# A fused convolution and two expert layers on one core: GpSimd takes two of the weight splits, and a factor of 2 pi changes its place

## The chip, the cores and the metric

The kernel runs on one core of one Trainium2 chip. TensorE multiplies, VectorE (DVE) and ScalarE (ACT) work on tiles in SBUF and PSUM, GpSimd (POOL) does nothing but four small constants in this kernel, and SyncE issues nearly all the DMAs. The metric is device microseconds of one execution. Before the change the median of three runs is 2252.99 us (2252.92 to 2253.04).

## The reference, cut to what matters

```python
w = exp(weight - max);  w = w / (sum(w) + 1e-9)                 # 8 heads, 7 taps
out = np.einsum('hk,bskhg->bshg', w, x_unf)                     # causal 7-tap filter, 4 x 4096 tokens, 192 channels
h = x @ w_in;  g = h * np.cos(h);  x = g @ w_out                # layer one, 192 -> 2048 -> 192
h = np.maximum(x @ w_in, 0.0);  return h * h @ w_out            # layer two, the same sizes
```

Everything is float32 in and out.

## The kernel before, in words

The 16384 tokens are worked in 32 tiles of 512. For each tile VectorE makes the seven taps (`conv`), TensorE multiplies up from 192 channels to 2048 (`h`, in pairs of 128 rows, so eight pairs per tile and layer), ScalarE and VectorE make the activation `g`, and TensorE multiplies down into `y`. Layer one is called A, layer two B. A turn `i` of the program has 16 slots: the eight pairs of A of tile `i` and the eight of B of tile `i - 1`, in the order of the table `SLOTS` (the first turn has only the A pairs, `FIRST_SLOTS`). In each slot TensorE does the up products of that slot's pair together with the down products of the pair four slots earlier (`LAG`).

Each factor is split into a high part, rounded to the multiplier's format, and a low part that holds the rest: three products (low by high, high by low, high by high) stand for one of float32. So the weights too exist as `_hi` and `_lo`. High parts are written by ScalarE (`down_hi_main`, L514, and `down_hi_side`, L518, for the down weights), low parts by VectorE by subtracting the high part from the staged float32 weights (L663 for layer one, L678 for layer two). The staged down weights of both layers lie in one buffer, `late`, one after the other: the second layer's load waits until the first layer's low parts are made. 128 of the 192 output channels are the main ones (`dn_hi`, `dn_lo`), 64 the side ones (`dn_side`, which holds both parts).

Layer one's `h` is divided by 2 pi when it is read (L528), so that the cosine can be taken of turns: L686 and L688 take off the whole turns, L537 is the sine with a quarter turn added, L694 multiplies. What is missing, a factor of 2 pi, is in the down weights of layer one: `scale=TWO_PI` at L514 and L518, and the multiplication in L663.

Which instruction stands where is written by hand. In the first turn VectorE does `layer1_down_lo` in slots 3 and 4 (its pairs A0 and A1), ScalarE the high parts in the same slots; the tables `LATE_AT` and `LATE_LOW_AT` put the second layer's weights at later slots: ScalarE's `dn_hi_B` at slot 8 of the first turn, VectorE's `dn_lo_B` and `dn_side_B` at slot 2 of the second turn. TensorE waits for low parts before the first down products of A (`down_waits`), and for those of B a turn later. `FILL` puts eight products on zeros before two of the first turn's last down steps.

`read_y1` (L554, L555, ScalarE) and `split_y1` (L729 to L738, VectorE) read `y_A` from PSUM once per tile and make layer two's input of it.

Of the kernel before, what the change touches and what calls it, by code (L numbers as in the profile page):

```python
# [17 lines left out]
ALU = mybir.AluOpType  # L18
ACT = mybir.ActivationFunctionType
F32 = mybir.dt.float32  # L20
# [3 lines left out]
P = 128  # L24
# [93 lines left out]
def tile_program(nc, x, taps_in, w1i, w1o, w2i, w2o, out):  # L118
# [15 lines left out]
    with ExitStack() as ctx:  # L134
# [72 lines left out]
        wi_lo = sem("wi_lo")  # L207
        late_hi_made = sem("late_hi_made")
        late_lo = sem("late_lo")
        even_made = sem("even_made")  # L210


# [41 lines left out]
        @block.sync  # L254
        def _(sp):
            def load_x(t):
                sp.dma_start(xt[:, :], x[t]).then_inc(x_loaded, 16)

            def load_layer1_up(part, a, b):
                sp.dma_start(stage_in[:, a:b], w1i[0:P, a:b]).then_inc(wi_loaded[part], 16)  # L260
                for half in (top, low):
                    sp.dma_start(stage_in_side[half, a:b], w1i[P:D, a:b]).then_inc(wi_loaded[part], 16)

            def store_y(t):
                sp.wait_ge(y2_copied, t + 1)
                sp.dma_start(out_tiles[t, 0:P, :], yt).then_inc(y_stored, 16)
                sp.wait_ge(y2_summed, t + 1)
                sp.dma_start(out_tiles[t, P:D, :], yt_side).then_inc(y_stored, 16)

            def load_layer2_up(half):  # L270
                cols = slice(half * HALF, (half + 1) * HALF)
                sp.dma_start(stage_main, w2i[0:P, cols]).then_inc(up2_loaded, 16)
                for rows in (top, low):
                    sp.dma_start(stage_side[rows, :], w2i[P:D, cols]).then_inc(up2_loaded, 16)

            def load_down(weights):
                sp.dma_start(stage_out, weights.rearrange("p (c d) -> p c d", d=D)).then_inc(down_loaded, 16)

            load_x(0)
            load_layer1_up(0, 0, FIRST_PART)  # L280
            load_layer1_up(1, FIRST_PART, F)
            load_down(w1o)
            sp.wait_ge(tap_done, K)
            load_x(1)
            sp.wait_ge(wi_lo, 4)
            load_layer2_up(0)
            sp.wait_ge(late_lo, 2)
            load_down(w2o)
            sp.wait_ge(tap_done, 2 * K)
            load_x(2)  # L290
            sp.wait_ge(late_lo, 4)
            sp.wait_ge(even_made, 1)
            load_layer2_up(1)

            sp.wait_ge(tap_done, 3 * K)
            load_x(3)
            for i in (2, 3):
                store_y(i - 2)
                sp.wait_ge(tap_done, (i + 2) * K)
                load_x(i + 2)  # L300
            with sp.Fori(4, TILES - 2) as i:
                store_y(sp.snap(i - 2))
                sp.wait_ge(tap_done, sp.snap((i + 2) * K))
                load_x(sp.snap(i + 2))
            for t in range(TILES - 4, TILES):
                store_y(t)
            sp.wait_ge(y_stored, 32 * TILES)

        @block.tensor
        def _(pe):  # L310
# [4 lines left out]
            def up_waits(turn, s, kind, p):  # L315
                freed = turn.before(s, HB)
                if freed:
                    pe.wait_ge(taken[freed[0]], freed[1])
                if p == 0 and kind == "A":
                    pe.wait_ge(x1_hi, 3 * (turn.i + 1))  # L320
                    pe.wait_ge(x1_made, turn.i + 1)
                if p == 0 and kind == "B":
                    pe.wait_ge(x2_made, turn.i)
                if turn.peeled and turn.i == 0 and p in (0, 2):
                    pe.wait_ge(wi_lo, 2 + p)
                if turn.peeled and turn.i == 1 and p == 0 and kind == "B":
                    pe.wait_ge(late_lo, 4)
                    pe.wait_ge(even_made, 1)
                if turn.peeled and turn.i == 1 and p == NP // 2 and kind == "B":
                    pe.wait_ge(late_lo, 8)  # L330
                    pe.wait_ge(even_made, 2)

            def up_step(turn, s, kind, p, rows, k):
# [26 lines left out]

            def down_waits(turn, kind, p, back):
                if turn.peeled and turn.i - back == 0 and p == 0:
                    pe.wait_ge(late_lo, 2)
                if turn.peeled and turn.i - back == 1 and p == 0 and kind == "B":
                    pe.wait_ge(late_lo, 6)
                if kind == "B" and p == 0 and turn.runs("O") and not turn.last(kind, back):
                    pe.wait_ge(y2_copied, turn.i - 1)
                    pe.wait_ge(y2_summed, turn.i - 1)
                if fine(turn, p):
                    pe.wait_ge(hi_made[kind], turn.count(kind, p, back))  # L370
                else:
                    pe.wait_ge(lo_made[kind], turn.count(kind, p, back))
# [109 lines left out]
        def _(act):  # L482
# [26 lines left out]
                act.activation(up_even[hi_rows["B"], half, :], even[:, :, 0, :], ACT.Copy).then_inc(even_made, 1)  # L509

            def down_hi_main(k):

                act.wait_ge(down_loaded, {"A": 16, "B": 32}[k])
                act.activation(dn_hi[k][:, :, :], stage_out[:, :, 0:P], ACT.Copy,  # L514
                               scale={"A": TWO_PI, "B": 1.0}[k]).then_inc(late_hi_made, 1)

            def down_hi_side(k):
                act.activation(dn_side[k][:, :, 0:SIDE], stage_out[:, :, P:D], ACT.Copy,  # L518
                               scale={"A": TWO_PI, "B": 1.0}[k]).then_inc(late_hi_made, 1)

            def read_h(turn, s, kind, p):
                act.wait_ge(filled[kind], turn.count(kind, p))
# [24 lines left out]
            def read_y1(turn, back):  # L547

                act.wait_ge(down_low["A"][0], turn.count("A", NP - 1, back))
                act.wait_ge(down_top["A"][1], turn.count("A", NP - 1, back))  # L550
                if back and turn.runs("B", 1):
                    act.wait_ge(filled["B"], turn.count("B", NP - 1, 1))
                x_hi = layer_in(turn, "B", back - 1)[0]
                act.activation(y_side[top, :], y["A"][low, 1, :], ACT.Copy).then_inc(y1_copied, 1)  # L554
                act.activation(x_hi[:, :], y["A"][:, 0, :], ACT.Copy).then_inc(y1_copied, 1)  # L555

            def read_y2(turn):
                count = turn.count("B", NP - 1, 1)
# [69 lines left out]
        def _(dve):  # L628
# [25 lines left out]
                dve.tensor_tensor(up_lo["A"][:, a:b], stage_in[:, a:b], up_hi["A"][:, a:b].bitcast(F32),  # L654
                                  ALU.subtract).then_inc(wi_lo, 1)

            def layer1_down_lo(m):
                dve.wait_ge(late_hi_made, m + 1)
                if m == 0:
                    lo, staged, hi = dn_lo["A"][:, :, :], stage_out[:, :, 0:P], dn_hi["A"][:, :, :]  # L660
                else:
                    lo, staged, hi = dn_side["A"][:, :, SIDE:], stage_out[:, :, P:D], dn_side["A"][:, :, 0:SIDE]
                dve.scalar_tensor_tensor(out=lo, in0=staged, scalar=TWO_PI, in1=hi.bitcast(F32), op0=ALU.mult,  # L663
                                         op1=ALU.subtract).then_inc(late_lo, 1)

            def late_lo_part(n):
                if n in (1, 3):
                    cols = slice(n // 2 * HALF, (n // 2 + 1) * HALF)
                    parts = ((up_lo["B"][:, cols], stage_main, up_hi["B"][:, cols]),
                             (up_side["B"][hi_rows["B"], cols], stage_side[hi_rows["B"], :],  # L670
                              up_side["B"][hi_rows["B"], cols]))
                else:
                    parts = ((dn_lo["B"][:, :, :], stage_out[:, :, 0:P], dn_hi["B"][:, :, :]),
                             (dn_side["B"][:, :, SIDE:], stage_out[:, :, P:D], dn_side["B"][:, :, 0:SIDE]))
                for m, (lo, staged, hi) in enumerate(parts):

                    dve.wait_ge(late_hi_made, 2 * n + 1 + m)
                    dve.tensor_tensor(lo, staged, hi.bitcast(F32), ALU.subtract).then_inc(late_lo, 1)  # L678

            def fraction(turn, r, p):  # L680
# [44 lines left out]
            def split_y1(turn, back):  # L725
                n = turn.i + 1 - back
                x_hi, x_lo, x_side, x_side_lo = layer_in(turn, "B", back - 1)
                dve.wait_ge(y1_copied, n * 2 - 1)
                dve.tensor_tensor(y_side[top, :], y["A"][top, 1, :], y_side[top, :], ALU.add)\  # L729
                   .then_inc(x2_step, 1)  # L730
                dve.wait_ge(x2_step, n * 2 - 1)
                dve.tensor_copy(x_side[low, :], y_side[top, :])
                dve.tensor_copy(x_side[top, :], y_side[top, :]).then_inc(x2_step, 1)
                dve.wait_ge(y1_copied, n * 2)
                dve.tensor_tensor(x_lo[:, :], y["A"][:, 0, :], x_hi[:, :].bitcast(F32),
                                  ALU.subtract)
                dve.wait_ge(x2_step, n * 2)
                dve.tensor_tensor(x_side_lo[lo_rows["B"], :], y_side[top, :],  # L738
                                  x_side[top, :].bitcast(F32), ALU.subtract).then_inc(x2_made, 1)
# [8 lines left out]
            def body(turn):  # L748
# [10 lines left out]
                for s, (kind, p) in enumerate(turn.slots()):  # L759
# [16 lines left out]
                            tap(turn, k)  # L776
                    if kind == "A" and turn.runs("A"):
                        fraction(turn, s % RING, p)
                    if turn.peeled and turn.i == 0 and kind == "A" and p < 2:
                        layer1_down_lo(p)  # L780
                    if turn.peeled and (turn.i, s) in LATE_LOW_AT:
                        late_lo_part(LATE_LOW_AT[turn.i, s])

            turns(dve, body)


# [40 lines left out]
```

## Time and profile before

| | |
|---|---|
| median of 3 runs | 2252.99 us |
| the profiled execution | 2253.41 us |
| its span | 2251.1 us |
| TensorE matmul busy | 2239.1 us (99%) |
| VectorE busy | 1774.6 us (79%) |
| ScalarE busy | 1734.8 us (77%) |
| GpSimd busy | 0.2 us, 4 instructions |
| mean granted TensorE clock | 0.999 |

The span runs from the first to the last instruction of the trace; 2.3 us of the profiled execution's time lie around it. Busy shares are means over the whole; TensorE is busy nearly all the time, so what matters is where in the program it is not, and what it waits for there. Chains and waits of the profile name for each instruction what released it last.

### The profile page before, as it was taken

What the parts mean: (1) busy time and instruction counts of PE and PEld (TensorE: products, weight loads), DVE (VectorE), ACT (ScalarE), POOL (GpSimd) and SP (SyncE); (2) the same over time, 40 slices, a digit from 0 to 9 for tenths busy, and PEclk for the clock granted to TensorE, in tenths of its full rate; (3) what the DMA queues carried; (4) which work ended last, traced back from release to release, by engine and by line L of the source; (5) the groups of instructions that cost most, each with busy time, mean ns of one, the idle gap of its engine ahead of it and who ended that gap; (6) DMA issues with size and microseconds to landing.
All of it is one profiled execution on the core that took longest, in us unless ns stands there. A gap on an engine that the chain in (4) does not pass through costs nothing.

```text
span 2251.1 us, 46857 instructions
## 1 busy us (share of the span) xinstructions
PE 2239.1 (99%) x19526; PEld 2213.3 (98%) x19526; DVE 1774.6 (79%) x1813; ACT 1734.8 (77%) x1844; POOL 0.2 (0%) x4
## 2 busy tenths in 40 slices
PE   8999999999999999999999999999999999999999
PEld 7899999999999999999999999999999999999998
DVE  8887788777787777887778877778877788777773
ACT  6677777777877777777778777787777787777876
POOL 0000000000000000000000000000000000000000
PEclk9999999999999999999999999999999999999999
DMA  4000000000000000000000000000000000000000
GB/s 127 27 15 15 9 14 12 10 14 7 14 14 7 14 9 13 14 7 14 14 7 14 14 7 14 7 14 14 7 14 14 7 14 14 7 14 7 7 8 15
DMA packets 13456, 33.26 MB, mean 15 GB/s; under 512 B 1905, under 2 KB 1905, under 8 KB 13169
## 3 DMA queue, kind: packets, MB, share of 16 engines
q1 hardware_dynamic: 13280, 32.81, 4.9%
q8 instruction: 24, 0.39, 0.1%
q14 instruction: 8, 0.06, 0.0%
q10 hardware_dynamic: 144, 0.00, 0.0%
HBM read 20.22 MB, written 12.58 MB: 15 GB/s over the span
## 4 chain that ended last, share of the span: by engine, by line
PE 97%; DVE 2%; ACT 1%; issue 0%; DMA 0%
PE h L346 10%; PE h L350 10%; PE h L348 10%; PE h L352 10%; PE y_A L402 5%; PE y_A L396 5%; PE y_A L400 5%; PE y_A L398 5%; PE y_A L404 5%; PE h L355 5%; PE y_B L400 5%; PE y_B L398 5%; PE y_B L396 5%; PE y_B L404 5%; PE y_B L402 5%; DVE conv L712 0%
## 5 line engine op out<-in xcount | busy, mean ns | idle before, releaser
L698 DVE TENSOR_TENSOR g_lo<-g,g_hi 128x1024 fp32r<-128x1024 f32 x512 | 625.2, 1221 | 272.0 <-ACT g_hi L545 271.1
L545 ACT ACTIVATE g_hi<-g 128x1024 fp32r<-128x1024 f32 x512 | 538.3, 1052 | 44.1 <-DVE g L694 43.4
L537 ACT ACTIVATE w<-w,quarter 128x1024 f32<-128x1024 f32 x256 | 295.5, 1154 | 304.6 <-DVE w L688 304.6
L396 PE MATMUL y_A<-g_hi,dn_lo_A 64*128 64x512 f32 x1024 | 396.9, 388 | 0.1
L402 PE MATMUL y_A<-g_hi,dn_side_A 64*128 64x512 f32 x1024 | 396.3, 387 | 0.0
L398 PE MATMUL y_A<-g_hi,dn_hi_A 64*128 64x512 f32 x1024 | 396.0, 387 | 0.0
L400 PE MATMUL y_A<-g_lo,dn_hi_A 64*128 64x512 f32 x1024 | 395.8, 387 | 0.0
L404 PE MATMUL y_A<-g_lo,dn_side_A 64*128 64x512 f32 x1024 | 395.8, 387 | 0.0
L348 PE MATMUL h<-x_hi_A,up_lo_A 64*128 64x512 f32 x1024 | 394.5, 387 | 0.0
L352 PE MATMUL h<-x_hi_A,up_hi_A 64*128 64x512 f32 x1024 | 394.5, 386 | 0.0
L350 PE MATMUL h<-x_lo_A,up_hi_A 64*128 64x512 f32 x1024 | 394.4, 386 | 0.0
L396 PE MATMUL y_B<-g_hi,dn_lo_B 64*128 64x512 f32 x1000 | 386.6, 387 | 0.0
L398 PE MATMUL y_B<-g_hi,dn_hi_B 64*128 64x512 f32 x1000 | 386.1, 386 | 0.0
L400 PE MATMUL y_B<-g_lo,dn_hi_B 64*128 64x512 f32 x1000 | 386.0, 386 | 0.0
L404 PE MATMUL y_B<-g_lo,dn_side_B 64*128 64x512 f32 x992 | 382.9, 386 | 0.0
L402 PE MATMUL y_B<-g_hi,dn_side_B 64*128 64x512 f32 x992 | 382.9, 386 | 0.0
L352 PE MATMUL h<-x_hi_B,up_hi_B 64*128 64x512 f32 x992 | 382.9, 386 | 0.0
L348 PE MATMUL h<-x_hi_B,up_lo_B 64*128 64x512 f32 x992 | 382.9, 386 | 0.0
L350 PE MATMUL h<-x_lo_B,up_hi_B 64*128 64x512 f32 x992 | 382.9, 386 | 0.0
L694 DVE TENSOR_TENSOR g<-w,g 128x1024 f32<-128x1024 f32 x256 | 313.7, 1225 | 22.7 <-ACT w L537 1.2
L688 DVE SCALAR_TENSOR_TENSOR w<-w,g 128x1024 f32<-128x1024 f32 x256 | 313.7, 1225 | 8.8
L528 ACT ACTIVATE g<-h 128x1024 f32<-128x1024 f32 x256 | 262.2, 1024 | 70.2 <-PE h L352 59.5
(122 smaller groups left out, 6180.0 us busy)
## 6 DMA issues: line engine op xcount, KB each, us to landing
xt<-x SPq DMA_DIRECT2D x32, 393.0 KB, 3.1
out<-late SPq DMA_DIRECT2D x32, 256.0 KB, 2.0
out<-late SPq DMA_DIRECT2D x32, 128.0 KB, 2.3
late<-w_out SPq DMA_DIRECT2D x2, 1536.0 KB, 9.5
stage_in_side<-w_in SPq DMA_DIRECT2D x2, 512.0 KB, 4.2
stage_in_side<-w_in SPq DMA_DIRECT2D x4, 256.0 KB, 5.3
w<-w_in SPq DMA_DIRECT2D x1, 768.0 KB, 7.1
stage_in_side<-w_in SPq DMA_DIRECT2D x2, 384.0 KB, 9.1
```

Of the source, the lines that this page charges most:

```text
L348: mm = pe.matmul(dst, up_lo[kind][rows, f], x_hi[rows, :], start=False, stop=z)
L350: mm = pe.matmul(dst, up_hi[kind][rows, f], x_lo[rows, :], start=False, stop=z)
L352: mm = pe.matmul(dst, up_hi[kind][rows, f], x_hi[rows, :], start=False, stop=z)
L396: mm = pe.matmul(sums[:, 0, :], dn_lo[kind][rows, c, :], hi, start=a, stop=False)
L398: mm = pe.matmul(sums[:, 0, :], dn_hi[kind][rows, c, :], hi, start=False, stop=False)
L400: mm = pe.matmul(sums[:, 0, :], dn_hi[kind][rows, c, :], lo, start=False, stop=z)
L402: mm = pe.matmul(sums[:, 1, :], dn_side[kind][rows, c, :], hi, start=a, stop=False)
L404: mm = pe.matmul(sums[:, 1, :], dn_side[kind][rows, c, :], lo, start=False, stop=z)
L545: act.activation(g_hi[:, s % RING, :, :], g[:, s % RING, :, :], ACT.Copy).then_inc(hi_made[kind], 1)
L688: dve.scalar_tensor_tensor(out=v, in0=v, scalar=ROUND, in1=u, op0=ALU.subtract, op1=ALU.subtract).then_inc(frac, 1)
L694: dve.tensor_tensor(u, v, u, ALU.mult).then_inc(g_made, 1)
L698: dve.tensor_tensor(g_lo[:, r, :, :], g[:, r, :, :], g_hi[:, r, :, :].bitcast(F32), ALU.subtract).then_inc(lo_made[kind], 1)
```

## The change

GpSimd gets a program of two subtractions, the low parts of the main channels of the down weights: `dn_lo_A` as soon as ScalarE has made `dn_hi_A`, `dn_lo_B` as soon as it has made `dn_hi_B`. VectorE no longer does them. A new semaphore `pool_lo` counts them, and the three places that waited for VectorE's `late_lo` wait for both. The 2 pi leaves the down weights of layer one and is applied where `y_A` is read: as a scale in ScalarE's two reads, and in VectorE's two instructions that read `y_A` from PSUM, which turn from `tensor_tensor` into `scalar_tensor_tensor`.

```diff
+        pool_lo = sem("pool_lo")
...
-            sp.wait_ge(late_lo, 2)
+            sp.wait_ge(late_lo, 1)
+            sp.wait_ge(pool_lo, 1)
             load_down(w2o)
...
                 if turn.peeled and turn.i - back == 0 and p == 0:
-                    pe.wait_ge(late_lo, 2)
+                    pe.wait_ge(late_lo, 1)
+                    pe.wait_ge(pool_lo, 1)
                 if turn.peeled and turn.i - back == 1 and p == 0 and kind == "B":
-                    pe.wait_ge(late_lo, 6)
+                    pe.wait_ge(late_lo, 4)
+                    pe.wait_ge(pool_lo, 2)
...
-                act.activation(dn_hi[k][:, :, :], stage_out[:, :, 0:P], ACT.Copy,
-                               scale={"A": TWO_PI, "B": 1.0}[k]).then_inc(late_hi_made, 1)
+                act.activation(dn_hi[k][:, :, :], stage_out[:, :, 0:P], ACT.Copy).then_inc(late_hi_made, 1)
...
-                act.activation(y_side[top, :], y["A"][low, 1, :], ACT.Copy).then_inc(y1_copied, 1)
-                act.activation(x_hi[:, :], y["A"][:, 0, :], ACT.Copy).then_inc(y1_copied, 1)
+                act.activation(y_side[top, :], y["A"][low, 1, :], ACT.Copy, scale=TWO_PI).then_inc(y1_copied, 1)
+                act.activation(x_hi[:, :], y["A"][:, 0, :], ACT.Copy, scale=TWO_PI).then_inc(y1_copied, 1)
...
-                dve.scalar_tensor_tensor(out=lo, in0=staged, scalar=TWO_PI, in1=hi.bitcast(F32), op0=ALU.mult,
-                                         op1=ALU.subtract).then_inc(late_lo, 1)
+                dve.tensor_tensor(dn_side["A"][:, :, SIDE:], stage_out[:, :, P:D],
+                                  dn_side["A"][:, :, 0:SIDE].bitcast(F32), ALU.subtract).then_inc(late_lo, 1)
...
-                dve.tensor_tensor(y_side[top, :], y["A"][top, 1, :], y_side[top, :], ALU.add)\
-                   .then_inc(x2_step, 1)
+                dve.scalar_tensor_tensor(out=y_side[top, :], in0=y["A"][top, 1, :], scalar=TWO_PI, in1=y_side[top, :],
+                                         op0=ALU.mult, op1=ALU.add).then_inc(x2_step, 1)
...
-                dve.tensor_tensor(x_lo[:, :], y["A"][:, 0, :], x_hi[:, :].bitcast(F32),
-                                  ALU.subtract)
+                dve.scalar_tensor_tensor(out=x_lo[:, :], in0=y["A"][:, 0, :], scalar=TWO_PI,
+                                         in1=x_hi[:, :].bitcast(F32), op0=ALU.mult, op1=ALU.subtract)
...
+        @block.gpsimd
+        def _(pool):
+            for k, made in (("A", 1), ("B", 5)):
+                pool.wait_ge(late_hi_made, made)
+                pool.tensor_tensor(dn_lo[k][:, :, :], stage_out[:, :, 0:P], dn_hi[k][:, :, :].bitcast(F32),
+                                   ALU.subtract).then_inc(pool_lo, 1)
```

VectorE, slots 3 to 5 of the first turn, before (each name is output, then inputs; `late` holds the staged down weights):

```order
L686 TENSOR_SCALAR w<-g 128x1024
L688 SCALAR_TENSOR_TENSOR w<-w,g 128x1024
L663 SCALAR_TENSOR_TENSOR dn_lo_A<-late,dn_hi_A 128x2048
L694 TENSOR_TENSOR g<-w,g 128x1024
L708 TENSOR_SCALAR conv<-xt,taps 128x768
L686 TENSOR_SCALAR w<-g 128x1024
L688 SCALAR_TENSOR_TENSOR w<-w,g 128x1024
L663 SCALAR_TENSOR_TENSOR dn_side_A<-late,dn_side_A 128x16x64
L698 TENSOR_TENSOR g_lo<-g,g_hi 128x1024
```

And the same place after the change:

```order
L683 TENSOR_SCALAR w<-g 128x1024
L685 SCALAR_TENSOR_TENSOR w<-w,g 128x1024
L691 TENSOR_TENSOR g<-w,g 128x1024
L705 TENSOR_SCALAR conv<-xt,taps 128x768
L683 TENSOR_SCALAR w<-g 128x1024
L685 SCALAR_TENSOR_TENSOR w<-w,g 128x1024
L661 TENSOR_TENSOR dn_side_A<-late,dn_side_A 128x16x64
L695 TENSOR_TENSOR g_lo<-g,g_hi 128x1024
```

One instruction has gone, the one on 128x2048, ahead of the first product with the cosine; the order of the others is as it was.

VectorE, slot 2 of the second turn, before:

```order
L694 TENSOR_TENSOR g<-w,g 128x1024 [waits cosine]
L678 TENSOR_TENSOR dn_lo_B<-late,dn_hi_B 128x2048 [waits late_hi_made]
L678 TENSOR_TENSOR dn_side_B<-late,dn_side_B 128x16x64 [waits late_hi_made]
L698 TENSOR_TENSOR g_lo<-g,g_hi 128x1024 [waits hi_made_A]
L686 TENSOR_SCALAR w<-g 128x1024 [waits taken_A]
```

After:

```order
L691 TENSOR_TENSOR g<-w,g 128x1024 [waits cosine]
L675 TENSOR_TENSOR dn_side_B<-late,dn_side_B 128x16x64 [waits late_hi_made]
L695 TENSOR_TENSOR g_lo<-g,g_hi 128x1024 [waits hi_made_A]
L683 TENSOR_SCALAR w<-g 128x1024 [waits taken_A]
L685 SCALAR_TENSOR_TENSOR w<-w,g 128x1024 [waits whole]
```

Here too the one on 128x2048 has gone.

GpSimd, its whole program after the change (before it ended with the fourth of the constants):

```order
L821 MEMSET const-float32-0.0 128x1
L821 MEMSET const-float32-1.0 128x1
L821 MEMSET const-bfloat16-1.0 128x1
L821 MEMSET const-uint8-127 128x1
L783 UNCONDITIONAL_BRANCH [waits barrier_Pool_Activation_PE_DVE_SP_gather]
L788 ISA
L788 TENSOR_TENSOR dn_lo_A<-late,dn_hi_A 128x2048 [waits late_hi_made]
L788 TENSOR_TENSOR dn_lo_B<-late,dn_hi_B 128x2048 [waits late_hi_made]
```

The second subtraction waits for the fifth high part, `dn_hi_B`, which ScalarE makes in slot 8 of the first turn: it stands some eight slots earlier in the program than VectorE's did.

## Rows read from the trace of the kernel before

**Rows 1.** The page's first part: busy time, share, instructions.

```profile
PE 2239.1 (99%) x19526; PEld 2213.3 (98%) x19526; DVE 1774.6 (79%) x1813; ACT 1734.8 (77%) x1844; POOL 0.2 (0%) x4
```

**Rows 2.** Waits after 82.1 us: engine, line, releaser: total us, times, longest.

```profile
ACT w L537 <- DVE w L688: 292.9, 245, 3.6
...
PE h L346 <- ACT g L530: 0.7, 1, 0.7
```

**Rows 3.** The chain that ended last, 16 to 50 us: start, us, what.

```profile
22.88 1.28 DVE dn_lo_A L663
...
24.99 1.22 DVE g L694
...
46.94 1.01 ACT g L528
...
48.00 0.50 PE h L346
```

**Rows 4.** VectorE in order of time, 16 to 83 us: start, us, what, idle before it.

```profile
21.65 1.23 DVE L688 SCALAR_TENSOR_TENSOR w<-w,g 128x1024 f32<-128x1024 f32 x1
22.79 2.29 DVE L663 SCALAR_TENSOR_TENSOR dn_lo_A<-late,dn_hi_A 128x2048 fp32r<-128x2048 f32 x1
...
30.05 1.22 DVE L698 TENSOR_TENSOR g_lo<-g,g_hi 128x1024 fp32r<-128x1024 f32 x1
...
51.00 1.22 DVE L698 TENSOR_TENSOR g_lo<-g,g_hi 128x1024 fp32r<-128x1024 f32 x1
...
56.24 1.22 DVE L698 TENSOR_TENSOR g_lo<-g,g_hi 128x1024 fp32r<-128x1024 f32 x1
...
82.20 2.29 DVE L678 TENSOR_TENSOR dn_lo_B<-late,dn_hi_B 128x2048 fp32r<-128x2048 f32 x1
```

**Rows 5.** ScalarE in order of time, 20 to 50 us.

```profile
20.52 1.90 ACT L514 ACTIVATE dn_hi_A<-late 128x2048 fp32r<-128x2048 f32 x1
22.91 1.15 ACT L537 ACTIVATE w<-w,quarter 128x1024 f32<-128x1024 f32 x1 [0.49 <-DVE w L688]
...
47.84 1.91 ACT L514 ACTIVATE dn_hi_B<-late 128x2048 fp32r<-128x2048 f32 x1
```

**Rows 6.** TensorE matmuls in order of time, 28 to 82 us.

```profile
28.24 0.39 PE L352 MATMUL h<-x_hi_A,up_hi_A 64*128 64x512 f32 x1
31.41 0.46 PE L346 MATMUL h<-x_side_lo,up_side_A 64*128 64x512 f32 x1 [2.79 <-DVE g_lo L698]
...
52.45 0.39 PE L396 MATMUL y_A<-g_hi,dn_lo_A 64*128 64x512 f32 x1
...
61.06 2.12 PE L455 MATMUL y_B<-x_side_last 128*128 128x512 f32 x8
...
66.09 0.39 PE L400 MATMUL y_A<-g_lo,dn_hi_A 64*128 64x512 f32 x1
66.64 0.47 PE L396 MATMUL y_A<-g_hi,dn_lo_A 64*128 64x512 f32 x1
...
82.00 0.50 PE L346 MATMUL h<-x_side_B,up_side_B 64*128 64x512 f32 x1 [0.70 <-ACT g L530]
```

**Rows 7.** TensorE by stretches: us, busy (matmuls), granted clock, DMA share, GB/s.

```profile
31.40:32.40 1.00, 0.99 (x8) 0.98 0.68 209
32.40:35.50 3.10, 3.10 (x17) 0.50 0.94 392
```

**Rows 8.** Groups by shape: line, operation, shapes, count, busy us, mean ns, idle before.

```profile
L729 DVE TENSOR_TENSOR y_side<-y_A,y_side 64x512 f32<-64x512 f32 x32 | 21.8, 682 | 99.5 <-ACT y_side L554 99.5
...
L528 ACT ACTIVATE g<-h 128x1024 f32<-128x1024 f32 x256 | 262.2, 1024 | 70.2 <-PE h L352 59.5
L530 ACT ACTIVATE g<-h 128x1024 f32<-128x1024 f32 x256 | 260.9, 1019 | 61.3 <-PE h L355 55.4
```

**Rows 9.** One tile's reading in the steady part: VectorE's last step, TensorE's first use.

```profile
209.26 0.68 DVE L738 TENSOR_TENSOR x_side_lo<-y_side,x_side_B 64x512 fp32r<-64x512 f32 x1
...
211.73 0.39 PE L346 MATMUL h<-x_side_B,up_side_B 64*128 64x512 f32 x1
```

More of the change, by code:

```diff
@@ L290, in _ @@
             load_x(2)
-            sp.wait_ge(late_lo, 4)
+            sp.wait_ge(late_lo, 3)
             sp.wait_ge(even_made, 1)
@@ L326, in up_waits @@
                 if turn.peeled and turn.i == 1 and p == 0 and kind == "B":
-                    pe.wait_ge(late_lo, 4)
+                    pe.wait_ge(late_lo, 3)
                     pe.wait_ge(even_made, 1)
                 if turn.peeled and turn.i == 1 and p == NP // 2 and kind == "B":
-                    pe.wait_ge(late_lo, 8)
+                    pe.wait_ge(late_lo, 6)
                     pe.wait_ge(even_made, 2)
@@ L513, in down_hi_main @@
                 act.wait_ge(down_loaded, {"A": 16, "B": 32}[k])
-                act.activation(dn_hi[k][:, :, :], stage_out[:, :, 0:P], ACT.Copy,
-                               scale={"A": TWO_PI, "B": 1.0}[k]).then_inc(late_hi_made, 1)
+                act.activation(dn_hi[k][:, :, :], stage_out[:, :, 0:P], ACT.Copy).then_inc(late_hi_made, 1)
             def down_hi_side(k):
-                act.activation(dn_side[k][:, :, 0:SIDE], stage_out[:, :, P:D], ACT.Copy,
-                               scale={"A": TWO_PI, "B": 1.0}[k]).then_inc(late_hi_made, 1)
+                act.activation(dn_side[k][:, :, 0:SIDE], stage_out[:, :, P:D], ACT.Copy).then_inc(late_hi_made, 1)
             def read_h(turn, s, kind, p):
@@ L655, in layer1_up_lo, with layer1_down_lo @@
                                   ALU.subtract).then_inc(wi_lo, 1)
[L657 to L662, printed above, removed]
-                dve.scalar_tensor_tensor(out=lo, in0=staged, scalar=TWO_PI, in1=hi.bitcast(F32), op0=ALU.mult,
-                                         op1=ALU.subtract).then_inc(late_lo, 1)
+            def layer1_down_lo():
+                dve.wait_ge(late_hi_made, 2)
+                dve.tensor_tensor(dn_side["A"][:, :, SIDE:], stage_out[:, :, P:D],
+                                  dn_side["A"][:, :, 0:SIDE].bitcast(F32), ALU.subtract).then_inc(late_lo, 1)
             def late_lo_part(n):
@@ L672, in late_lo_part @@
                 else:
-                    parts = ((dn_lo["B"][:, :, :], stage_out[:, :, 0:P], dn_hi["B"][:, :, :]),
-                             (dn_side["B"][:, :, SIDE:], stage_out[:, :, P:D], dn_side["B"][:, :, 0:SIDE]))
+                    parts = ((dn_side["B"][:, :, SIDE:], stage_out[:, :, P:D], dn_side["B"][:, :, 0:SIDE]),)
                 for m, (lo, staged, hi) in enumerate(parts):
-                    dve.wait_ge(late_hi_made, 2 * n + 1 + m)
+                    dve.wait_ge(late_hi_made, 2 * n + 1 + m + (n == 2))
                     dve.tensor_tensor(lo, staged, hi.bitcast(F32), ALU.subtract).then_inc(late_lo, 1)
@@ L778, in body @@
                         fraction(turn, s % RING, p)
-                    if turn.peeled and turn.i == 0 and kind == "A" and p < 2:
-                        layer1_down_lo(p)
+                    if turn.peeled and turn.i == 0 and kind == "A" and p == 1:
+                        layer1_down_lo()
                     if turn.peeled and (turn.i, s) in LATE_LOW_AT:
```

## The prediction

> **What bounds the kernel now.** I read the page's busy shares first, then the waits, the chain, and the first 90 us in order of time. TensorE is busy in 2239.1 of 2251.1 us [rows 1], so only work that TensorE waits for can matter. After 82.1 us the list of waits has one matmul wait, 0.7 us (the instruction at 82.00); all other waits there are of VectorE and ScalarE, above all 292.9 us of ScalarE for VectorE [rows 2]. That is slack: from 82.00 us the end is 82.00 plus TensorE's own work, and the change takes none of it away. The price is therefore read as the shift of that instruction.
>
> Before it, VectorE leads. The chain runs through VectorE's pair stream: `w` ends at 22.88, `dn_lo_A` follows, the cosine product starts at 24.99, and by way of the sine and the read of `h` it comes out at TensorE's slot at 48.00 [rows 3]. VectorE stands idle once between 21 and 60 us, for 0.26 us by my reading of its whole list; the rows kept are in [rows 4]. TensorE sits idle from 28.6 to 31.4, until the first `g_lo` [rows 6]. From 48.00 to 72 TensorE and VectorE run nearly in step: a `g_lo` comes every 5.24 us (51.00, 56.24) [rows 4], and TensorE's slot plus its eight products on zeros lasts as long. The down step alone that starts at 52.45 needs the `g_lo` that ends at 52.22: slack 0.23 us [rows 4, 6].
>
> **The change, part by part.**
>
> *`dn_lo_A` leaves VectorE.* The instruction lasts 2.29 us, but the next one, the cosine product, needs the sine, which ends at 22.91 + 1.15 = 24.06 [rows 5]. It can move from 24.99 to 24.1 at best: a gain of 0.9 us, and the wait for the sine is what is late next. All that follows on VectorE is in the same order, so the slot at 48.00 comes 0.9 us earlier.
>
> *`dn_lo_B` leaves VectorE.* It stood at 82.20 [rows 4], behind the last point where TensorE waits. The instructions behind it come sooner, and nobody waits for them: 0.
>
> *GpSimd's subtraction, alone.* No row shows GpSimd on a large tile. From below: VectorE's 2.29 us for the same shape [rows 4], one pass. From above: three passes, two reads and a write one after the other, 6.87 us. I take two passes, 4.58 us, since the instruction has two large inputs. The Trainium skill (GPSIMD Engine Reference, section 3.1) gives 4.497 us for this operation and size; with it each term below is 0.1 us smaller. As a mere producer GpSimd is in time: `dn_hi_A` is done at 20.52 + 1.90 = 22.42 [rows 5], and TensorE and the load of the second down weights need the result only behind the first `g_lo`, at 31.3 before and 30.4 with the gain. Even 6.87 us would end at 29.3. `dn_lo_B` starts after `dn_hi_B`, at 49.75, and is needed at about 91: 40 us of cover. If the first subtraction took over 8 us, that cover would be gone and TensorE would wait for `pool_lo`.
>
> *GpSimd beside VectorE.* The trace has no stretch with both at work in SBUF, so the ends are: fully beside each other (0 us), and fully one after the other, a VectorE instruction with two SBUF tiles waiting out the whole subtraction. I take the second end. It is the choice that decides the sign. The Trainium skill (SBUF — State Buffer, section Who interferes with whom) says that GpSimd reads through an interface which VectorE's second SBUF input also uses, and that whichever starts first blocks the other for its whole instruction; no run here shows it yet. By that rule the sum is the one that follows; without it the change is worth the 0.9 us.
>
> With exclusion, place by place. First subtraction: `w` (two inputs) is under way until 22.88, then VectorE would be waiting for the sine, so GpSimd gets in at 22.9 and ends at 22.9 + 4.58 = 27.5. The cosine product starts there and not at 24.99: +2.5 us, on the chain to 48.00. Everything queued behind it on VectorE moves with it, the first `g_lo` (30.05) [rows 4] and so the load of the second down weights too, which has ten microseconds to spare before `dn_hi_B` at 47.84 [rows 5]. Second subtraction: ready at 49.75 (+2.5), in the middle of VectorE's full stretch. It gets in between two of its instructions and holds up the `g_lo` of 51.00, or one of the next, by 4.58 us. TensorE's slack there is 0.23 [rows 4, 6]: +4.35 us. VectorE cannot catch up, since the products on zeros and its own 5.24 us period leave nothing.
>
> *The clock.* After the idle 2.8 us TensorE was granted 0.50, the 1.2 GHz level, from 32.4 to 35.5 [rows 6, 7], so 3.1 us gave half the work, and with the edges 1.6 us are lost. There it cost nothing: TensorE had slack in that slot. In the second stall TensorE stands 4.3 us and I expect the same drop, now where it and VectorE run in step. Slack before the last down step: 66.09 plus the cadence of 0.23 against 66.64, 0.3 us [rows 6]. So +1.3 us; from below 0, if the clock holds.
>
> *The 2 pi at the reading of y.* ScalarE's read with a scale costs what one without does (L528 1024 ns with 1/2 pi, L530 1019 without) [rows 8], and on SBUF tiles VectorE's two forms last the same (L663 and L678, 2.29 us each) [rows 4]. From PSUM the trace has only the plain form, 682 ns [rows 8]; between 0 and twice as long for two instructions is 0 to 1.4 us per tile. I take 0. In the steady part the reading ends at 209.94, and TensorE uses it at 211.73 [rows 9]: 1.8 us of cover hide even the upper end. Without that cover it would be 32 times the excess.
>
> **The sum.** 2.5 + 4.35 + 1.3 = 8.2 us. Against the profiled execution's own 2253.41 us (a span of 2251.1 and 2.3 around it) that is 2261.6, and against the median, 0.4 lower, 2261.2. I say 2261. With 2.29 us for the subtraction the terms are 0.2, 2.1 and 0 to 1.3: 2255.3 to 2256.6. With 6.87: 4.8, 6.65 and 1.3: 2265.7.
>
> **The rivals.**
>
> *No contention.* GpSimd works beside VectorE; only the 0.9 us of the first part show: 2252.1. Not slower. For it: the two engines are separate in every row, and the time VectorE waits for ScalarE (24.06 is fixed) bounds the gain. Against it: both read the same tile types from the same SBUF at the moment when VectorE runs without a pause. It decides from an overlap at which the cosine product starts before 24.99.
>
> *Sharing.* Both go on, each slowed. The first subtraction then overlaps VectorE from 24.06 to 27.5; at half speed VectorE loses 1.7 of that, less the 0.9: +0.8. The second costs half of 4.58, less 0.23: +2.1. Together 2255.9, too little to tell from no change. For it: memory traffic is often shared; against it: nothing in the trace has that shape.
>
> *GpSimd is too slow.* Over 8 us each, TensorE waits for `pool_lo`; with exclusion at 9 us the terms are 6.9, 8.8 and 1.3: 2270.
>
> *The change doesn't do what it says.* The work is the same and the instructions are in the program; I give that no chance.
>
> **How the numbers follow.** Exclusion 0.60, its own range 2256 to 2266; no contention 0.24; sharing 0.13; too slow 0.03. What a measurement can tell from no change is 0.2%, 4.5 us. A gain of 4.5 us would need five times the best the chain offers: faster 0.02. Same: 0.24 + 0.13, and 0.05 of the exclusion case with a short subtraction, less the 0.02: 0.40. Slower: 0.58. The range goes from just under the rival without contention to 2264, which leaves out the 0.02 and about 0.13 above.
>
> **What would show it.** In the changed profile: GpSimd's two subtractions with their durations near 4.6 us, the first from 22.9; a gap on VectorE ahead of the cosine product until the first one ends, or a cosine product at 24.1; a gap of the second one's length on VectorE near 52 to 60 us; TensorE idle in front of the down step after the slot at 50.5, and a granted clock of 0.5 behind it; the instruction that stood at 82.00 at about 90. The forecast is wrong if VectorE's instructions start during a subtraction, or if GpSimd's lasts under 3 us or over 7.

## The result, and the profile after

The changed kernel takes 2262.89 us (median of 6, 2260.59 to 2264.56) against 2253.01 us before (6 runs): a ratio of 1.0042, 95% interval 1.0032 to 1.0051. It is slower by 9.9 us; forecast were 2261 and a range of 2251.8 to 2264. The profiled execution took 2264.56 us, the longest of the six and above that range; its span is 2261.6, 10.5 more than before.

GpSimd's two subtractions in the changed kernel, in order of time (start, us, instruction, idle before it and releaser):

```profile
22.99 4.62 POOL L788 TENSOR_TENSOR dn_lo_A<-late,dn_hi_A 128x2048 fp32r<-128x2048 f32 x1 [22.54 <-ACT dn_hi_A L517]
52.30 4.57 POOL L788 TENSOR_TENSOR dn_lo_B<-late,dn_hi_B 128x2048 fp32r<-128x2048 f32 x1 [24.69 <-ACT dn_hi_B L517]
```

And VectorE beside them, same columns:

```profile
21.94 1.23 DVE L685 SCALAR_TENSOR_TENSOR w<-w,g 128x1024 f32<-128x1024 f32 x1
24.39 4.30 DVE L691 TENSOR_TENSOR g<-w,g 128x1024 f32<-128x1024 f32 x1 [1.22 <-ACT w L538]
...
32.53 1.22 DVE L695 TENSOR_TENSOR g_lo<-g,g_hi 128x1024 fp32r<-128x1024 f32 x1
...
52.33 5.62 DVE L685 SCALAR_TENSOR_TENSOR w<-w,g 128x1024 f32<-128x1024 f32 x1
57.88 1.21 DVE L695 TENSOR_TENSOR g_lo<-g,g_hi 128x1024 fp32r<-128x1024 f32 x1
```

The two VectorE instructions that start while a subtraction runs are not late in starting; they are long. Both last 1.22 us elsewhere (their groups mean 1237 and 1242 ns with these two in it; 1225 and 1225 before). The first ends at 28.69, 1.08 us after GpSimd's end at 27.61; the second at 57.95, 1.08 us after 56.87. So each did its work only once GpSimd had ended. (The second subtraction starts at 52.30, where VectorE's own stood at 82.20: 30 us earlier, ten places of the slot table and not the eight that the part on the change has.) A stall on VectorE looks like busy time here: the lists of waits show nothing of it, and VectorE's busy sum has grown by 3.4 us (1774.6 to 1778.0) though 4.6 us of work left it.

TensorE, the places that answer to [rows 6] (at 59.14 the down step that stood at 52.45):

```profile
33.89 0.76 PE L348 MATMUL h<-x_side_lo,up_side_A 64*128 64x512 f32 x1 [4.97 <-DVE g_lo L695]
...
50.46 0.50 PE L348 MATMUL h<-x_side_lo,up_side_A 64*128 64x512 f32 x1 [0.73 <-ACT g L529]
...
59.14 0.79 PE L400 MATMUL y_A<-g_hi,dn_lo_A 64*128 64x512 f32 x1 [4.08 <-DVE g_lo L695]
...
77.38 0.46 PE L400 MATMUL y_A<-g_hi,dn_lo_A 64*128 64x512 f32 x1
...
92.75 0.50 PE L348 MATMUL h<-x_side_B,up_side_B 64*128 64x512 f32 x1 [0.70 <-ACT g L531]
```

The slot at 82.00 and 92.75 is the last place where TensorE waits. Against before, the slot at 48.00 is 2.46 us late, the down step at 52.45 6.69 us, the last down step at 66.64 10.74 us, and the instruction at 82.00 10.75 us. Behind it nothing moves any more: the list of waits after 91 us has, as in [rows 2], one matmul wait of 0.7 us. What came between 59.14 and 77.38 is the clock (columns: stretch, us, busy (matmuls), granted clock, DMA share, GB/s):

```profile
54.00:58.00 4.00, 1.06 (x10) 1.00 0.00 0
58.00:69.00 11.00, 9.86 (x32) 0.53 0.12 33
69.00:80.00 11.00, 10.85 (x68) 1.00 0.16 51
```

TensorE was granted half its speed, 1.2 of 2.4 GHz, in nearly the whole stretch from 58 to 69. In stretches of half a microsecond the grant falls at 58.0, 1.1 us before the 4.1 us of idling end, and is back at 68.3: 10.2 us. In [rows 7] the stretch shown at half was 3.1 us; read as finely it is 3.4 us.

The reading of y, with the 2 pi, answers to [rows 8] (group by shape, mean ns):

```profile
L726 DVE SCALAR_TENSOR_TENSOR y_side<-y_A,y_side 64x512 f32<-64x512 f32 x32 | 21.8, 682 | 103.4 <-ACT y_side L556 103.4
```

682 ns as before.

### The profile page after: what moved, and what is told of

Same layout as the page of the kernel before. It is cut to its first block, busy times and chain, and to the rows that moved or that the text cites. A ratio compares the mean times of both kernels' runs of the same rounds, so it can differ in the third digit from the quotient of the medians.

```text
span 2261.6 us, 46862 instructions
## 1 busy us (share of the span) xinstructions
PE 2243.6 (99%) x19526; PEld 2214.7 (98%) x19526; DVE 1778.0 (79%) x1811; ACT 1735.2 (77%) x1844; POOL 9.4 (0%) x6
## 4 chain that ended last, share of the span: by engine, by line
PE 98%; DVE 1%; ACT 1%; issue 0%; DVEq 0%
PE h L348 10%; PE h L352 10%; PE h L354 10%; PE h L350 10%; PE y_A L400 5%; PE y_A L402 5%; PE y_A L406 5%; PE y_A L404 5%; PE y_A L408 5%; PE h L357 5%; PE y_B L404 5%; PE y_B L402 5%; PE y_B L400 5%; PE y_B L406 5%; PE y_B L408 5%; PE y_B L459 1%
## 5 line engine op out<-in xcount | busy, mean ns | idle before, releaser
L691 DVE TENSOR_TENSOR g<-w,g 128x1024 f32<-128x1024 f32 x256 | 316.8, 1237 | 23.9 <-ACT w L538 2.4
L685 DVE SCALAR_TENSOR_TENSOR w<-w,g 128x1024 f32<-128x1024 f32 x256 | 318.0, 1242 | 8.8
```

Source lines behind the costliest of these rows:

```text
L685: dve.scalar_tensor_tensor(out=v, in0=v, scalar=ROUND, in1=u, op0=ALU.subtract, op1=ALU.subtract).then_inc(frac, 1)
L691: dve.tensor_tensor(u, v, u, ALU.mult).then_inc(g_made, 1)
```

## The experiments

Theory: GpSimd's instruction and VectorE's exclude each other in SBUF for the length of an instruction, and the stall that this makes on TensorE costs its clock. Rivals: the 2 pi costs something; each subtraction costs the same wherever it stands; the later delay is VectorE's and not the clock's; any GpSimd work excludes, not only reading.

**Both subtractions back on VectorE, the 2 pi left where the change puts it.** The new helper stands in VectorE's program; GpSimd's block is gone.

```diff
+            def main_lo(k, made):
+                dve.wait_ge(late_hi_made, made)
+                dve.tensor_tensor(dn_lo[k][:, :, :], stage_out[:, :, 0:P], dn_hi[k][:, :, :].bitcast(F32),
+                                  ALU.subtract).then_inc(pool_lo, 1)
...
+                    if turn.peeled and turn.i == 0 and kind == "A" and p == 0:
+                        main_lo("A", 1)
...
+                    if turn.peeled and (turn.i, s) == (1, 2):
+                        main_lo("B", 5)
```

> The changed kernel with both subtractions given back to VectorE at their old places; the 2 pi stays at the reading of y. Exclusion theory (GpSimd's subtractions hold VectorE up, the 2 pi costs nothing): 2253 us, ratio to before 1.000 within 0.1%, TensorE's slot at 48.0 and the last wait at 82.0. Rival (the 2 pi at the reading costs part of the 10 us): 2255 us or more, and VectorE's reads of y longer than 682 ns.

Measured: 2253.1 us (10 runs) against 2253.28, ratio 1.0000 (0.9990 to 1.0009); the slot at 48.05, the last wait at 82.14. VectorE's read of `y_A` lasts 683 ns, as before. The 2 pi is free within this noise, and the loss is with GpSimd.

**The first subtraction alone on GpSimd.** VectorE makes the second at its old place, in the helper of the first experiment (not shown again).

```diff
-            for k, made in (("A", 1), ("B", 5)):
+            for k, made in (("A", 1),):
```

> GpSimd makes only the first subtraction, VectorE the second at its old place. Exclusion: +2.5 us alone, 2255.5 us; slot at 50.5, down step at 55.0 and the last wait at 84.5 all moved by the same 2.5, and the clock's half stretch near 31 to 38 us costs nothing. Rival (each subtraction costs half of the 10 us, whatever stands there): +5 us, 2258.

Measured: 2255.44 us, ratio 1.0009 (1.0000 to 1.0019), so 2.2 us by the medians, with an interval that reaches 1; the trace carries the reading. TensorE in order of time:

```profile
33.65 0.76 PE L348 MATMUL h<-x_side_lo,up_side_A 64*128 64x512 f32 x1 [4.98 <-DVE g_lo L700]
...
50.23 0.50 PE L348 MATMUL h<-x_side_lo,up_side_A 64*128 64x512 f32 x1 [0.74 <-ACT g L529]
...
84.23 0.50 PE L348 MATMUL h<-x_side_B,up_side_B 64*128 64x512 f32 x1 [0.72 <-ACT g L531]
```

2.23 us late at both the slot and the last wait, as VectorE is. "Half of the 10 us each", 5 us, doesn't hold. A stall of 5 us with half the clock behind it (0.50 from 33.4 to 36.8 us) adds nothing at this place, since the slot at 50.23 waits for VectorE and ScalarE.

**The second subtraction alone on GpSimd.** VectorE makes the first.

```diff
-            for k, made in (("A", 1), ("B", 5)):
+            for k, made in (("B", 5),):
```

> GpSimd makes only the second subtraction, VectorE the first at its old place. Exclusion and clock: +4.2 us from the stall of the down step at 52.45 and +4 from the half clock behind it, 2261 us; the last wait at 90. Rival (no clock term): +4.2, 2257. Rival (half each): +5, 2258.

Measured: 2260.03 us (2258.38 to 2261.99), ratio 1.0028 (1.0018 to 1.0038). In the profiled execution (2260.44 us):

```profile
48.33 0.50 PE L348 MATMUL h<-x_side_lo,up_side_A 64*128 64x512 f32 x1 [0.63 <-ACT g L529]
...
57.00 0.50 PE L400 MATMUL y_A<-g_hi,dn_lo_A 64*128 64x512 f32 x1 [4.07 <-DVE g_lo L700]
...
89.53 0.49 PE L348 MATMUL h<-x_side_B,up_side_B 64*128 64x512 f32 x1 [0.70 <-ACT g L531]
```

0.33 us late at the slot (before the subtraction begins; TensorE is as late at 31.75, against 31.41 before, so this comes from the start of the program), 4.22 more at the down step, 2.98 more at the last wait: the stall as read, and a clock term of 3 us. The clock, TensorE alone (us, busy (matmuls), granted clock, DMA share, GB/s):

```profile
58.00:64.90 6.90, 6.90 (x21) 0.51 0.00 0
64.90:80.00 15.10, 14.95 (x94) 1.00 0.34 97
```

The half stretch is 6.8 us here, after the same stall (4.07 us) that was followed by 10.2 us in the changed kernel. "No clock term" (2257) doesn't hold in this execution, and no run is below 2258.38. But four of the ten runs lie at 2258.4 to 2258.6, with mean clocks of 0.998 and 0.999, the profiled one and five others at 2259.6 to 2262.0, with 0.996 and 0.997: the clock term is not one number. The 2.2 and the 6.7 us of the two runs add up to 8.9 of the 9.9.

**Products on zeros in the stall.** The changed kernel, with TensorE kept at work where it would stand.

```diff
-WARM_UP, FILL = (42, 12), {5: 8, 6: 8}
+WARM_UP, FILL = (42, 12), {4: 16, 5: 8, 6: 8}
```

> The changed kernel with 16 products on zeros ahead of the down step that stalls (8 take 2.05 us, so 16 take 4.1 of its 4.2 us), so that TensorE is never idle there. Clock theory: the granted clock stays 1.00 from 52 to 80, the half stretch from 58 to 69 is gone and with it 4 us: 2259 us or less against the changed kernel's 2263, the last wait at 88.8. Rival (the later 4 us are VectorE's own delay and not the clock's): no gain, 2263, or slower.

Measured: 2259.29 us (2259.02 to 2259.71), ratio to before 1.0025 (1.0015 to 1.0035); 3.6 us less than the changed kernel by the medians, compared across runs. The same stretches as above:

```profile
54.00:58.00 4.00, 4.00 (x22) 1.00 0.00 0
58.00:69.00 11.00, 10.76 (x58) 1.00 0.12 37
69.00:80.00 11.00, 10.85 (x75) 1.00 0.18 54
```

and the last wait is at 88.53 instead of 92.75. The half stretch from 58 us is gone and 4.2 us with it (0.2 of them were there at the slot before, 50.24 against 50.46), while VectorE's long instructions are still there (4.30 and 5.65 us). That shows the clock term by itself, 4.0 us: the expected 2259 and 88.8 came to 2259.29 and 88.53. What is left, 6.5 us at the last wait, is what VectorE was held up.

**GpSimd only writes.** VectorE makes both subtractions, in the first experiment's form, and waits for `pool_done` before the second. GpSimd does nothing else.

```diff
+            pool.wait_ge(late_hi_made, 5)
+            pool.memset(dn_lo["B"][:, :, :].bitcast(F32), 0.0).then_inc(pool_done, 1)
```

> VectorE makes both subtractions at their old places. GpSimd only writes at the place of the second one: a memset of the same 128x2048 tile, which VectorE overwrites later. If the exclusion is over reading SBUF: VectorE's instructions beside the memset keep their 1.22 us, 2253 us, no change. Rival (any GpSimd work in SBUF holds VectorE up): the scalar_tensor_tensor beside it is longer by the memset's time, and the run slower by that and the half clock.

Measured: 2253.28 us, ratio 1.0001 (0.9991 to 1.0010). GpSimd, and VectorE beside it:

```profile
49.55 1.82 POOL L798 MEMSET dn_lo_B<- 128x2048 f32 x1 [49.10 <-ACT dn_hi_B L518]
```

```profile
49.60 1.23 DVE L693 SCALAR_TENSOR_TENSOR w<-w,g 128x1024 f32<-128x1024 f32 x1
50.75 1.22 DVE L703 TENSOR_TENSOR g_lo<-g,g_hi 128x1024 fp32r<-128x1024 f32 x1
```

Neither of the two is longer: a GpSimd instruction that only writes SBUF holds VectorE up in nothing that the trace shows.

**GpSimd reads one tile.** The same with a copy.

```diff
+            pool.tensor_copy(dn_lo["B"][:, :, :], dn_hi["B"][:, :, :].bitcast(F32)).then_inc(pool_done, 1)
```

> As the run with the memset, but GpSimd copies dn_hi_B into dn_lo_B (one SBUF input), which VectorE overwrites later. If reading is what excludes: VectorE's two-input instruction waits out the copy, whatever it lasts (2 to 3 us for one input), and the last wait moves by that less 0.2, plus a half clock stretch if TensorE's stall is long enough for one. Rival (only a GpSimd instruction with two inputs excludes): no VectorE instruction is longer than 1.3 us there, 2253 us.

Measured once, so the time has no interval and only the trace counts: 2254.85 us. GpSimd, then VectorE:

```profile
50.15 1.90 POOL L798 CAST dn_lo_B<-dn_hi_B 128x2048 fp32r<-128x2048 f32 x1 [49.70 <-ACT dn_hi_B L518]
```

```profile
50.21 2.92 DVE L693 SCALAR_TENSOR_TENSOR w<-w,g 128x1024 f32<-128x1024 f32 x1
```

The copy ends at 52.05 and VectorE's instruction at 53.13, again 1.08 us later. A memset of nearly the same length did nothing to the same instruction. So it is GpSimd's reading that excludes, with one input as with two. TensorE stalls 1.36 us here, its clock stays at 1.00 behind that stall, and the last wait is at 83.90, 1.56 us beyond the 0.34 that this run is already late at the slot before.

**The second subtraction in eight pieces.** The changed kernel otherwise.

```diff
+                for c in (range(0, NC, 2) if k == "B" else (None,)):
+                    cs = slice(0, NC) if c is None else slice(c, c + 2)
+                    op = pool.tensor_tensor(dn_lo[k][:, cs, :], stage_out[:, cs, 0:P], dn_hi[k][:, cs, :].bitcast(F32),
+                                            ALU.subtract)
+                    if c in (None, NC - 2):
+                        op.then_inc(pool_lo, 1)
```

> The changed kernel with the second subtraction cut in 8 pieces of 128x256, first to last from the same point. If the exclusion holds per instruction: VectorE gets in between pieces, so its instructions are each longer by one piece (0.6 to 0.7 us) over some eight of them, TensorE's stall is cut into short ones, the clock stays 1.00, and of the 10 us the 4 of the clock come back: 2258 to 2260 us. Rival (GpSimd keeps SBUF over its whole queue of pieces): one VectorE instruction of 5.5 us and 2263, as the changed kernel.

Measured: 2261.21 us (5 runs, 2259.32 to 2261.36), ratio 1.0034 (1.0020 to 1.0048); above the range I gave, though two of five lie in it, the profiled one (2259.55) among them. GpSimd's eight pieces (first start and the sum), then VectorE:

```profile
52.53 11.68 POOL L790 TENSOR_TENSOR dn_lo_B<-late,dn_hi_B 128x256 fp32r<-128x256 f32 x8 [24.68 <-ACT dn_hi_B L517]
```

```profile
52.56 1.80 DVE L685 SCALAR_TENSOR_TENSOR w<-w,g 128x1024 f32<-128x1024 f32 x1
54.28 1.76 DVE L695 TENSOR_TENSOR g_lo<-g,g_hi 128x1024 fp32r<-128x1024 f32 x1
55.96 1.75 DVE L691 TENSOR_TENSOR g<-w,g 128x1024 f32<-128x1024 f32 x1
57.63 1.49 DVE L709 SCALAR_TENSOR_TENSOR conv<-xt,taps,conv 128x768 f32<-128x768 f32 x1
59.05 1.22 DVE L683 TENSOR_SCALAR w<-g 128x1024 f32<-128x1024 f32 x1
```

The engines take turns, instruction by instruction: eight of VectorE's are longer, by 0.4 to 0.6 us each, the one-input `TENSOR_SCALAR` too (1.22 against 0.69), and the pieces now last 1.46 us each, with VectorE's turn in them. Cutting up shares VectorE's loss out and hardly reduces it: 4.1 us over the eight against 4.4 us (5.62 for 1.22) in one piece. TensorE's stall is two, of 0.8 and 2.15 us, and in the profiled execution the clock stays at 1.00 behind them:

```profile
54.00:69.00 15.00, 12.08 (x68) 1.00 0.09 27
```

The last wait is at 88.12 there, 6.1 us late. By the medians this version loses 8.0 us where the changed kernel loses 9.9; the two intervals overlap, so a gain by the cutting isn't shown. The three slower runs had a mean clock of 0.997 against this one's 0.998; no trace shows where they lost it.

**The second subtraction later.** The first stays on VectorE, and GpSimd waits for the ninth low part of layer one, near 81 us.

```diff
-            for k, made in (("A", 1), ("B", 5)):
+            for k, made in (("B", 5),):
                 pool.wait_ge(late_hi_made, made)
+                pool.wait_ge(lo_made["A"], 9)
```

> Only the second subtraction on GpSimd, and it waits for VectorE's ninth low part of layer one (at 81.0 us before), where TensorE is hardly ever held up. Exclusion, read by itself: VectorE has 4.6 us taken there and 2.3 given back, so a net 2.3; TensorE has the down step at 86.4 waiting for a low part that was ready at 86.8 in its middle, so it stalls up to 2.5 us, too short for the clock: 2253 to 2256 us. Rival (the subtraction costs what it cost at 52 us wherever it stands): 2260.

Measured: 2255.52 us, ratio 1.0011 (1.0001 to 1.0020), 2.3 us by the medians. GpSimd, VectorE, TensorE:

```profile
81.05 5.64 POOL L796 TENSOR_TENSOR dn_lo_B<-late,dn_hi_B 128x2048 fp32r<-128x2048 f32 x1 [80.61 <-DVE g_lo L700]
```

```profile
80.98 1.23 DVE L696 TENSOR_TENSOR g<-w,g 128x1024 f32<-128x1024 f32 x1
82.13 5.65 DVE L680 TENSOR_TENSOR dn_side_B<-late,dn_side_B 128x1024 fp32r<-128x1024 f32 x1
```

```profile
88.97 0.50 PE L404 MATMUL y_A<-g_lo,dn_hi_A 64*128 64x512 f32 x1 [1.73 <-DVE g_lo L700]
```

Here VectorE's product (80.98) had begun first, and GpSimd's subtraction beside it is long: 5.64 us for 4.57. VectorE's next instruction, begun while GpSimd's is under way, is long in turn (5.65 us for 1.22). Whoever is second waits. TensorE stalls 1.73 us, with the clock at 1.00 behind it; its wait at 82.00 has not moved (81.92). The place decides the price, 2.3 us here and 6.7 at 50 us; even this place, the cheapest tried for this subtraction, is not a gain, because GpSimd needs 4.6 us of what VectorE needs 2.3.

**ScalarE instead of GpSimd.** The kernel before; in the first turn only, the next tile's first tap moves from VectorE to ScalarE, after `dn_side_A`.

```diff
+            def first_tap(turn):
+                act.wait_ge(x_loaded, (turn.i + 2) * 16)
+                act.wait_ge(x1_made, turn.i + 1)
+                act.activation(conv_parts, parts[:, :, 0:HALF_TOK], ACT.Copy, scale=taps[:, 0:1]).then_inc(tap_done, 1)
```

> The kernel before, with nothing on GpSimd; in the first turn alone the first tap of the next tile (1.01 us on VectorE at 26.13) is made by ScalarE, which waits for VectorE there anyway. If what GpSimd cost is exclusion and VectorE's stretch from 21 to 60 us is the bound as read: ScalarE's work beside VectorE lengthens nothing, VectorE has 0.93 us less, the slot at 48.00 and the last wait at 82.0 come 0.9 us earlier, 2252.1 us against 2253.0. Rival (the 2 us stretches elsewhere, as the down steps on zeros, give it back): the slot at 47.1, but the last wait at 82.0 and 2253.0. Rival (ScalarE is late with the read of h or the high part): slower than before by up to 1 us.

The edit also takes that tap out of VectorE's program.

Measured: 2252.28 us (11 runs) against 2253.23 (15 runs), ratio 0.9996 (0.9987 to 1.0005). The interval holds 1, so the runs alone don't tell the gain; the trace has it at each milestone. ScalarE, then VectorE, then TensorE:

```profile
25.88 0.93 ACT L574 ACTIVATE conv<-xt,taps 128x768 f32<-128x768 f32 x1
```

```profile
25.05 1.22 DVE L701 TENSOR_TENSOR g<-w,g 128x1024 f32<-128x1024 f32 x1
26.19 0.69 DVE L693 TENSOR_SCALAR w<-g 128x1024 f32<-128x1024 f32 x1
```

```profile
47.13 0.50 PE L346 MATMUL h<-x_side_lo,up_side_A 64*128 64x512 f32 x1 [0.69 <-ACT g L528]
...
81.13 0.50 PE L346 MATMUL h<-x_side_B,up_side_B 64*128 64x512 f32 x1 [0.69 <-ACT g L530]
```

0.87 us earlier at both, and no VectorE instruction beside ScalarE's is longer. The median lies 0.04% below the kernel before, which is not shown to be more than noise.

## Why the prediction was right, and where its size was off

*What bounds the kernel.* Right: the shift of the instruction at 82.00 (10.75 us) is all of the change of the span (10.5), and the ScalarE experiment shows the same link from the other side.

*GpSimd alone.* I took 4.58 us between 2.29 and 6.87; it was 4.62 and 4.57. Two passes was a choice between bounds, and that it came within 0.04 us is in part luck: the copy, with one input, lasts 1.90 us and not the 2.29 of a pass, and twice that is 3.8. The Trainium skill's 4.497 us (GPSIMD Engine Reference, section 3.1) lies 0.1 below, and the trace decides.

*Beside VectorE.* The choice that decided the sign was right. The traces agree with the rule of the Trainium skill (SBUF — State Buffer, section Who interferes with whom): a reading GpSimd instruction excludes VectorE's two-input one (5.62 us for 1.22), a writing one doesn't (1.23), and the later of the two waits (5.64 us on GpSimd in the run with the late subtraction). The rival without contention falls by the same rows. So does sharing: at half speed a product that starts at 24.39 would have ended near 27, and it ended at 28.69, 1.08 us behind GpSimd. But the signs that I had named were wrong. "The forecast is wrong if VectorE's instructions start during a subtraction", and a cosine product that starts before 24.99 was to speak for no contention: both happened (24.39 and 52.33, beside subtractions from 22.99 and 52.30). A held-up instruction starts on time in the trace and lasts long, so the test has to be its end, not its start.

*The two terms.* 2.5 us for the first subtraction: 2.46 in the changed kernel, 2.23 alone. 4.35 us for the second: 4.23 and 4.22. (The 0.23 between the two runs is there before the stall: TensorE's last product ahead of it starts at 28.54 and 28.28.) The first `g_lo` moved by 2.48. GpSimd was in time as a producer: TensorE's waits in the trace are for `g_lo` and for ScalarE, none for `pool_lo`.

*The clock.* This is the term that was mis-sized: "So +1.3 us". I took the length of the half stretch from [rows 7], 3.1 us, as if it belonged to any stall; after the later stall it lasted 10.2 us, and cost 4.05 us in the changed kernel and 2.98 with the second subtraction alone, where it lasted 6.8. The experiment with products on zeros shows that this is the clock: 4.0 us came back with it. The term was 2.75 us too small; less the 0.16 by which the two terms above came out smaller, that is the difference between my 8.2 (8.15 unrounded) and the 10.75 at the last wait; against the medians, 8 expected and 9.9 measured. That the median lies inside the range is in part luck: the six runs spread over 4 us, and the profiled execution, with its 4.05 us, lies above the range. What sets the length of such a stretch stays open. The length of the stall alone doesn't set it: 2.8 us of idling was followed by 3.4 us at half before and by 6.8 us with the second subtraction alone, 5.0 us by 3.4 us with the first alone and by 6.8 us in the changed kernel.

*The 2 pi.* 0, as taken: 682 ns in both forms, and 2253.1 us with it alone.

## What to carry to other kernels

A second engine relieves a busy one only if both can really run at once; here GpSimd reading SBUF held VectorE up until it had ended, so that moving 2.3 us of work off VectorE put 4.4 us on it where it had no idle time. Such a stall hides in the profile as a long instruction, not as a wait: compare single durations with the group's mean before you believe busy shares. Price a stall of TensorE by itself and by the clock behind it, and ask at each place whether the engine has slack for either: 5 us of standing at 30 us of this kernel added nothing to VectorE's 2.2 to 2.5, and 4 us at 55 cost 8 with the clock.

## What was not expected of the hardware

The one-input `TENSOR_SCALAR` of VectorE is held up as well as the two-input forms (1.22 against 0.69 us beside a piece of 128x256).

The stalls of TensorE and the clock behind them, as the traces have them: 1.36 us (the copy), 1.73 (the late subtraction) and 0.8 with 2.15 (the pieces), all behind 53 us, left it at 1.00 in those executions. The stall before the first `g_lo`, near 30 us, was followed by 0.50 in every execution profiled, even where it was only 1.87 us, in the ScalarE experiment:

```profile
30.55 0.47 PE L346 MATMUL h<-x_side_lo,up_side_A 64*128 64x512 f32 x1 [1.87 <-DVE g_lo L705]
```

```profile
32.00:35.00 3.00, 3.00 (x17) 0.50 0.86 356
```

So the length of the stall alone does not tell whether the clock falls: 1.87 us was followed by a fall and 2.15 us was not. Nor does it tell for how long. After 2.8 us at this place the half stretch was 3.4 us before and 6.8 us with the second subtraction alone; it can begin while TensorE still stands:

```profile
31.00:37.50 6.50, 5.75 (x28) 0.50 0.65 242
```

The longest, after 4.1 us, was 10.2 us.

The same program can lose a different amount in different runs: with the second subtraction alone the runs go from 2258.4 to 2262.0 us, with the mean clock between 0.999 and 0.996; with the stall filled they lie within 0.7 us.
